# Where VectorE makes four low parts of the last expert's down weights

## The reference

```python
def _moe2_ref(x, w_gate, w1, w2, capacity):       # x: 1536 x 384
    logits = x @ w_gate                           # 8 experts
    expert_idx = np.argmax(logits, axis=1)
    ...                                           # gate_w, and disp[e, slot] = x[i] for the tokens of e
    h = np.maximum(np.einsum('ecd,edf->ecf', disp, w1), 0.0)   # w1: 8 x 384 x 1024
    y = np.einsum('ecf,efd->ecd', h, w2)                        # w2: 8 x 1024 x 384
    ...                                           # out[i] = gate_w[i] * y[expert_idx[i], pos[i]]
```

## Time and profile before

| what | value |
|---|---|
| median of 3 runs | 420.84 us |
| the profiled execution, its own time | 420.92 us |
| its span (first to last instruction) | 419.2 us |
| PE busy | 403.1 us (96%) |
| DVE busy | 265.4 us (63%) |
| ACT busy | 191.4 us (46%) |
| POOL busy | 183.6 us (44%) |
| mean granted TensorE clock | 0.997 of full speed |

### The profile page before, as it was taken

One profiled execution on the slowest core, in us unless ns is written; L12 is line 12 of the kernel. 1 busy time (PEld: TensorE's weight loads), 2 busy tenths in 40 slices (PEclk: granted clock), 3 DMA queues, 4 the chain that ended last, 5 costly groups with the idle time before them and its releaser, 6 DMA issues.

```text
span 419.2 us, 9352 instructions
## 1 busy us (share of the span) xinstructions
PE 403.1 (96%) x3194; PEld 387.9 (93%) x3195; DVE 265.4 (63%) x571; ACT 191.4 (46%) x442; POOL 183.6 (44%) x191
## 2 busy tenths in 40 slices
PE   5799999999999999999999999999999999999992
PEld 5698899999999999999999999998999999999972
DVE  6898877664427434264333789582888797735990
ACT  2879955341221212211123333343859595626950
POOL 3999808554222442224435567253503031103252
PEclk9999999999999999999999999999999999999998
DMA  6997027436980000000100245316996694908500
GB/s 236 405 380 248 3 65 215 148 101 230 367 301 0 35 24 0 0 0 19 38 0 0 75 132 155 111 42 223 378 360 176 211 291 142 322 5 258 165 3 27
DMA packets 34329, 61.74 MB, mean 147 GB/s; under 512 B 4798, under 2 KB 27310, under 8 KB 34288
## 3 DMA queue, kind: packets, MB, share of 16 engines
q1 hardware_dynamic: 31280, 55.92, 39.7%
q0 software_dynamic: 3008, 5.29, 3.7%
HBM read 47.92 MB, written 15.18 MB: 151 GB/s over the span
## 4 chain that ended last, share of the span: by engine, by line
PE 86%; DVE 5%; issue 2%; POOL 2%; PEld 1%; ACT 1%; DMA 0%; POOLq 0%; DVEq 0%; PEldq 0%; ACTq 0%
PE bank L1436 24%; PE bank L1397 23%; PE bank L1619 8%; PE bank L1650 5%; PE bank L1670 4%; PE bank L1720 3%; PE bank L1381 3%; PE bank L1345 2%; PE bank L1373 2%; PE bank L1685 2%; PE bank L1537 2%; PE bank L1588 1%; PE bank L1331 1%; PE bank L1547 1%; PE bank L1445 1%
## 5 line engine op out<-in xcount | busy, mean ns | idle before, releaser
L553 POOL TENSOR_TENSOR g_low<-act_full,g_high 128x384 fp32r<-128x384 f32 x63 | 65.1, 1034 | 111.3 <-ACT g_high L697 111.2
L697 ACT ACTIVATE g_high<-act_full 128x384 fp32r<-128x384 f32 x64 | 33.7, 526 | 146.1 <-DVE act_full L1032 133.5
L1397 PE MATMUL bank<-x_split,w_high 128*128 (+1 forms) x384 | 98.6, 337 | 0.2 <-DVE w_low L945 0.2
L1026 DVE TENSOR_SCALAR neg<-bank,alpha_sb 128x384 f32<-128x384 f32 x64 | 39.4, 616 | 89.0 <-PE bank L1397 89.0
L1397 PEld LDWEIGHTS bank<-x_split,w_high 128*128 128x128 f32 x384 | 68.9, 188 | 0.9 <-DVE w_low L945 0.5
L611 POOL DMA_INDIRECT out<-y_out,token x24 | 30.9, 1289 | 86.2 <-ACT y_out L823 83.0
L1436 PE MATMUL bank<-w_high,g_high 128*128 128x384 f32 x189 | 64.5, 341 | 0.0
L1397 PE MATMUL bank<-x_split,w_low 128*128 (+1 forms) x192 | 64.4, 336 | 0.0
L1436 PE MATMUL bank<-w_high,g_low 128*128 128x384 f32 x189 | 63.8, 338 | 0.0
L1436 PE MATMUL bank<-w_low,g_high 128*128 128x384 f32 x189 | 63.8, 338 | 0.0
L1032 DVE SCALAR_TENSOR_TENSOR act_full<-bank,neg 128x384 f32<-128x384 f32 x64 | 35.7, 557 | 2.4
(11 more groups left out here) (171 smaller groups left out, 841.9 us busy)
## 6 DMA issues: line engine op xcount, KB each, us to landing
w_raw<-chunks SPq DMA_DIRECT2D x96, 192.0 KB, 5.9
w_raw<-chunks SPq DMA_DIRECT2D x32, 384.0 KB, 3.8
rk_in<-att_rk SPq DMA_DIRECT2D x12, 704.0 KB, 6.5
routed_rows<-fill SPq DMA_DIRECT2D x1, 5211.0 KB, 18.0
xe<-routed_rows SPq DMA_DIRECT2D x7, 579.0 KB, 5.4
v_in<-att_v SPq DMA_DIRECT2D x12, 200.0 KB, 6.3
out<-fill SPq DMA_DIRECT2D x1, 2304.0 KB, 23.3
x_split<-x_split POOLq DMA_DIRECT2D x18, 48.0 KB, 2.6
```

Of the source, the lines that this page charges most:

```text
L553: pool.tensor_tensor(gl[:, f % 4, :], act_full[:, f % 2, :], gh[:, f % 4, :].bitcast(f32), ALU.subtract).then_inc(s_gl, 1)
L697: act.activation(gh[:, f % 4, :], act_full[:, f % 2, :], ACT.Copy).then_inc(s_gh, 1)
L1026: dve.tensor_scalar(neg[:, f % 2, :], h, 0.0, alpha_sb[:, f:f + 1], ALU.min, ALU.mult)\
L1397: last = mm(bank[f % 4][:, 0:G], a[:, f, w], x[:, kc, bass.ds(g * G, G)], start=kc == 0 and i == 0, stop=kc == KC - 1 and i == 2)
```

## The change

Of the eight low parts of expert 7's down weights, f = 0 to 3 stay at the end of expert 6's branch. f = 4 and 5 are made in expert 7's branch behind the relu of half 0, f = 6 behind the relu of half 1, and f = 7 behind `flip_low` of half 0. The same number of instructions of each kind is run. In the `Else` branches of experts 6 and 7, f = 4 to 7 move in the same way from expert 6 to the places behind `relu_low` of f = 0 to 3 in expert 7; with these inputs both experts are of the other kind.

```diff
+                    def last_low2(*fs):
+                        for f in fs:
+                            if e == E - 1:
+                                split_low2(E - 1, f)
+
                     flip_relu(e, 0, 0)
                     if e == E - 2:
                         last_low1(0, 1, 2)
                     else:
                         low2(0)
+                    last_low2(4, 5)
                     flip_relu(e, 0, 1)
                     last_low1(3)
+                    last_low2(6)
                     flip_low(e, 0, 0)
+                    last_low2(7)
...
                     if e == E - 2:
-                        low2(0)
-                    low2(1, 2, 3, 4, 5, 6, 7)
+                        low2(0, 1, 2, 3)
+                    else:
+                        low2(1, 2, 3, 4, 5, 6, 7)
                 with dve.Else():
                     dve.sem_inc(s_fr[0], 2)
                     for f in range(NFE):
                         relu_low(e, f, 2 * P)
...
-                        if FIRST <= e + 1 < E:
+                        if FIRST <= e + 1 < E and not (e == E - 2 and f >= HF):
                             split_low2(e + 1, f)
+                        if e == E - 1 and f < HF:
+                            split_low2(e, HF + f)
```

## The result

| | before | after |
|---|---|---|
| runs | 22 | 22 |
| median | 420.89 us | 420.33 us |
| lowest | 420.65 us | 420.04 us |
| the profiled execution, its own time | 420.92 us | 420.33 us |
| its span | 419.2 us | 418.6 us |

Forecast were 419.9 us and a gain of 0.96. The median lies in the stated range of 419.5 to 420.8 and outside the 419.75 to 420.1 that the likeliest case had for itself.

The account below looks back on a forecast made before the run. TensorE, 96% busy, idles in expert 7 because relus queue behind weight low parts; starting the down product at 406.50, not 407.46, gains 0.96: 420.92 - 0.96 = 419.96, against the median 419.88, said as 419.9 us; range 419.5 to 420.8.

Parts of the forecast that it names:

- the likeliest case: Whole kernel: expert 7's down product starts 0.96 us earlier and this lasts to the end; 419.9 us, chance 0.68.
- Relu 0 is bound by the low parts ahead of it, and their pitch is 0.47 us: VectorE, expert 7: four low parts removed ahead of relu 0 save 1.88 us; relu 0 starts at 403.37 instead of 405.25.
- Two low parts fit between the relus, f = 6 and f = 7 lie under waits: VectorE, expert 7: the pair between the relus ends 0.35 us before half 1 is ready; nothing waits for f = 6.
- The covers: Expert 7's down product: spare time before `flip_low` 0, f = 4 to 7 and `flip_low` 1 are needed: 1.0, 1.1, 1.8 us.
- ScalarE's `flip_high` 0 is the later of the two paths, D = U + 5.57: U: expert 7's first up matmul; D: its down product's start, put at 406.50 by ScalarE, 406.34 by the second transposes.
- second half of rival 1: Expert 7: down product follows the second transposes by 0.88 us, not 0.35, starting at 406.87; gain 0.59; rival 1's chance 0.16.
- 407.46 is where the kernel before starts the down product: Expert 7, TensorE: start before the change, from which the forecast 406.50 was taken to give the gain of 0.96 us.
- 420.92 less the gain: Whole kernel: profiled execution before, 420.92 us, less 0.96 gives 419.96; against the median 419.88.
- rival 1: Expert 7: a scatter's port use delays the copies, relu 0 at 404.23, part of gain lost; gain 0.61, 420.2 us; chance 0.16.
- the 405.5 that I had named as a sign of being wrong: Expert 7, VectorE: relu 1 was forecast at 405.26; a start behind 405.5 would show the forecast wrong.
- Rival 3, the scatters: GpSimd's queue sets the end, its scatters held by VectorE's nearly gapless work; slower, 421.4 to 422.0 us; chance 0.05.
- the next scatters would be held by one or two low parts: GpSimd, expert 7: second scatter may be held by f = 4 and 5, ending 405.84, third by f = 6, ending 407.3.

Follow-up runs that it names:

- a_copy: The changed kernel, unchanged, timed and profiled once more in the first group; 420.35 us, ratio 0.9989 to the kernel before.
- not_made: Changed kernel, but expert 7's low parts f = 4 to 7 never made, VectorE only waiting and counting; 420.20 us, ratio 0.9982 to the kernel before.
- all_behind: Changed kernel with f = 4 to 7 all behind relu 1 and ahead of `flip_low` 0; 420.67 us, ratio 0.9994 to the kernel before.
- two_moved: Changed kernel, but six low parts stay ahead of relu 0, only f = 6 and 7 moved; 420.21 us, ratio 0.9977 to the kernel before.
- a_again: The changed kernel, unchanged, a third profile, in the third group; 420.25 us, ratio 0.9983 to the kernel before.
- one_moved: Changed kernel, but seven low parts stay ahead of relu 0, only f = 7 moved; 420.84 us, ratio 0.9990 to the kernel before.
- b_copy: The kernel before, unchanged, timed and profiled once more in the first group; 421.16 us, ratio 1.0004 to the kernel before.

## Why the prediction was right, and where it was not

- *Relu 0 is bound by the low parts ahead of it, and their pitch is 0.47 us.* Right. I forecast relu 0 2.02 us behind the first low part (403.37 - 401.35); it came 2.08 behind it in the profile after (403.47 - 401.39) and 2.02 in a_copy.
- *Two low parts fit between the relus, f = 6 and f = 7 lie under waits.* Right, and shown: not_made has the same D, and all_behind loses 0.51 us once the cover is used up. The covers themselves were loosely worked out: 1.62 us is how long the eight matmuls ran, while the next one started 1.46 behind their start (408.92 - 407.46 in the profile before), which makes the first cover 0.86 and not 1.0; and 1.1 and 1.8 don't follow from the times beside them. None of this reached the forecast. The prediction did not see that two moved would have sufficed, though its own numbers had it: a slack of 1.0 us ahead of the first transposes is two low parts.
- *ScalarE's `flip_high` 0 is the later of the two paths, D = U + 5.57.* Wrong in the path, and by 0.08 us in the sum. ScalarE's path was sized rightly, at U + 5.54: `flip_high` 0 ends at 406.63 in the profile after, and with the 0.10 that is 406.73. But D is 406.84. The other path was mis-sized: it took 0.35 us from expert 6 for the way from the second transposes to the down product, and here that way takes 0.58 (406.84 - 406.26). In expert 6 TensorE had not waited, nine other transposes stood ahead, and the loads of the four ran 0.11 ahead of their matmuls. Behind a wait, load and matmul start together, the four last 0.66 in place of 0.60, and the down product's first load comes 0.55 behind them in place of 0.32. The first transposes of expert 7 in two_moved had also waited and lasted 0.66; in the profile after they had not, and lasted 0.60. The second half of rival 1 asked about this distance, with 0.88 as its bound; the truth lay between.

ScalarE's `flip_high` 0 in the profile after, and TensorE's weight loads in expert 6 of the profile before and in expert 7 of the one after:

```profile
406.03 0.60 ACT L837 ACTIVATE expert_g_high<-bank 128x512 fp32r<-128x512 f32 x1 [3.50 <-PE bank L1752]
```

```profile
396.19 0.47 PEld L1741 LDWEIGHTS bank<-ident,expert_g_by_token 128*128 128x128 f32 x4
396.62 0.19 PEld L1670 LDWEIGHTS bank<-w_high,expert_g_high 128*128 128x128 f32 x1
```

```profile
406.25 0.42 PEld L1752 LDWEIGHTS bank<-ident,expert_g_by_token 128*128 128x128 f32 x4 [0.58 <-DVE expert_g_by_token L1213]
406.81 0.19 PEld L1681 LDWEIGHTS bank<-w_high,expert_g_high 128*128 128x128 f32 x1
```

- *407.46 is where the kernel before starts the down product.* True of that profile, but this was the term that failed most: it holds a delay that isn't always there. ScalarE's second `flip_high` in expert 6 started 0.95 us behind its transposes. Of the twelve profiles without added copies five have 0.88 to 0.97 and seven 0.71 or 0.72. In the kernel before VectorE sets D, so it pays: U + 6.53, 6.50 and 6.30 in its three profiles. In the changed one D is U + 5.65 in all three. The gain at this place is 0.65 to 0.88 us, and 0.96 took its upper end. The lowest times of one group agree: 420.86 to 420.06 where the delay stood, 420.64 to 420.02 where it didn't.
- *420.92 less the gain.* U moved by itself, 400.92 to 401.36 in the fourteen profiles, whatever the kernel. In the profile after its 0.26 came at the wait for the early rows' load at 264.93; in a_again it was there by 60 already. Between two single executions this is as large as a third of the effect: 0.88 - 0.26 - 0.03 behind D = 0.59, the difference of the two profiled executions.
- *The time.* 420.33 lies in the range because the range reaches over the rivals. The gain of 0.56 is nearer to the 0.59 to 0.61 of rival 1 than to 0.96, but that is a coincidence: the copies took 0.17 and 0.15 us and relu 0 started at 403.47, not at 404.23. Relu 1 started at 405.51, behind the 405.5 that I had named as a sign of being wrong; U was 0.26 late, and U + 4.32 is what I had forecast within 0.01.
- *Rival 3, the scatters.* The last scatter waited 1.40 us for ScalarE and not for its own queue. It did not decide. The forecast that the next scatters would be held by one or two low parts came true in a_copy and not in the profile after (below).

Not settled is why that `flip_high` is late on some occasions. Within the first group it was late in four of four profiles, in the second early in four of four, and in the third early in both without added copies; both kernels have had it late and early. So it seems to go with the occasion, or with the chip, which differed from group to group, rather than with the code. Nothing was varied that would make it come or go.

## What to carry to other kernels

Work out both bounds of a place, the one that is removed and the one that takes over, as a start relative to the same event of the bounding engine. The gain is their difference, and only as much work has to be moved as it takes to cross them; here two of the four.

A delay on an engine is paid in full by the version in which that engine sets the end and hardly by the other (0.51 and 0.10 us of 0.48, by the lowest times), so part of what such a change gains is its indifference to delays, and one profile of before may hold the worst or the best of them. Take a distance between two instructions from a row in which the engine had also just waited, not from one in full flow.

## What the runs showed that was not expected

In expert 7, a scatter on GpSimd that starts while VectorE runs four or more low parts without a gap ends about 0.86 us behind the run's end. Two rows, of two_moved and of the profile after:

```profile
402.36 2.76 POOL L611 DMA_INDIRECT out<-y_out,token  x1 [6.02 <-ACT y_out L823]
```

```profile
402.38 1.83 POOL L611 DMA_INDIRECT out<-y_out,token  x1 [5.76 <-ACT y_out L823]
404.51 0.97 POOL L611 DMA_INDIRECT out<-y_out,token  x1 [0.30 <-issue]
```

| low parts in the run | run ends | scatter ends | difference |
|---|---|---|---|
| 4 (after) | 403.35 | 404.21 | 0.86 |
| 6 (two_moved) | 404.26 | 405.12 | 0.86 |
| 7 (one_moved) | 405.08 | 405.93 | 0.85 |
| 8 (before) | 405.19 | 406.04 | 0.85 |

In these rows its duration is set by VectorE over a range of 1.83 to 3.69 us, against 0.97 alone. These are subtractions with both inputs in SBUF. The Trainium skill ("SBUF — State Buffer", "Who interferes with whom") infers that `tensor_tensor` does not hold up the writing of descriptors; beside it, it says that a VectorE instruction with two SBUF inputs does contend with a GpSimd instruction that reads SBUF. The four rows speak against the inference for these scatters, unless they fall under the second statement: they take their row numbers from the tile `token`, which lies in SBUF, and no run here separates the two.

It is not the run's length alone that decides. In the profile before, at 318.69, a scatter starts amid eight low parts of up weights and ends at 320.40, 0.25 us ahead of their end at 320.65. That run has a gap of 0.08 us behind its sixth low part, which ends at 319.55, and the scatter ends 0.85 behind that. Both rows are of the profile before:

```profile
316.65 4.00 DVE L1164 TENSOR_TENSOR w_low<-w_raw,w_high 128x384 fp32r<-128x384 f32 x8
```

```profile
318.69 1.71 POOL L611 DMA_INDIRECT out<-y_out,token  x1 [14.28 <-ACT y_out L823]
```

And two low parts can hold one as well. In a_copy the scatter of 404.43 ends at 405.78, 0.85 behind the end of the pair beside it, 404.93:

```profile
403.92 1.01 DVE L1157 TENSOR_TENSOR w_low<-w_raw,w_high 128x384 fp32r<-128x384 f32 x2
```

```profile
404.43 1.35 POOL L611 DMA_INDIRECT out<-y_out,token  x1 [0.31 <-issue]
```

In the profile after, the scatter of 404.51 starts beside the same pair (404.08, 1.03 us) and takes its 0.97. By the pitch of 0.47 it starts just ahead of the pair's second low part, and the one of a_copy just behind it. Nothing was varied that would show that this decides. Nor is a run without a gap always waited out: beside the six low parts that end at 379.04 the scatter of 378.18 took 1.71 us in the profile before and ended 0.85 behind them, while in b_copy the same scatter took 1.24 and ended 0.38 behind.
